# A routed feed-forward kernel in which half a tile of the first expert is placed inside the gating of the last dense tile, and the experts' products hold tokens still

## The reference

```
attention: 8 heads of 64, half of them with a local mask, half with a strided one
dense:     h = x @ w_in (512x2048);  g = h * sigmoid(1.702 h);  x = g @ w_out (2048x512)
routed:    out = x;  rows with x @ w_skip > 0 are computed, the others stay
           e = argmax(x @ w_gate)  (8 experts);  gate = softmax(...)[e]
           out[row] = x[row] + gate * (relu(x[row] @ w1[e]) @ w2[e])   (512x1024, 1024x512)
```

## Time and profile before

| | |
|---|---|
| median of 3 runs | 750.28 us (749.67 to 751.13) |
| profiled execution, its own time | 748.58 us |
| its span, first to last instruction | 747.0 us |
| mean granted TensorE clock | 0.967 of 2.4 GHz |
| TensorE busy | 687.1 us, 92% |
| VectorE, ScalarE, GpSimd busy | 401.9, 355.2, 151.8 us |

### The profile page before, as it was taken

One profiled execution on the slowest core, in us unless ns is written; L12 is line 12 of the kernel. 1 busy time (PEld: TensorE's weight loads), 2 busy tenths in 40 slices (PEclk: granted clock), 3 DMA queues, 4 the chain that ended last, 5 costly groups with the idle time before them and its releaser, 6 DMA issues.

```text
span 747.0 us, 15044 instructions
## 1 busy us (share of the span) xinstructions
PE 687.1 (92%) x4891; PEld 609.6 (82%) x4892; DVE 401.9 (54%) x1401; ACT 355.2 (48%) x1034; POOL 151.8 (20%) x200
## 2 busy tenths in 40 slices
PE   4799999999999999999999999999429999999992
PEld 3578888988888889888988889889329998888882
DVE  4767764474456334243342432523758685668854
ACT  5778765555655333333333332332326563456632
POOL 5345221213223002000010010100240333212331
PEclk9689999999999999999999999999859999999997
DMA  7647633224411502001020020100447686676751
GB/s 255 209 117 259 200 126 98 71 74 145 143 39 65 166 1 85 1 28 59 1 85 0 0 84 0 44 13 1 127 133 229 194 258 204 206 215 181 243 181 43
DMA packets 48455, 85.60 MB, mean 115 GB/s; under 512 B 7858, under 2 KB 11954, under 8 KB 48400
## 3 DMA queue, kind: packets, MB, share of 16 engines
q1 hardware_dynamic: 43664, 79.20, 33.3%
q0 software_dynamic: 3920, 4.65, 2.2%
q10 hardware_dynamic: 816, 1.05, 0.4%
HBM read 70.84 MB, written 18.52 MB: 120 GB/s over the span
## 4 chain that ended last, share of the span: by engine, by line
PE 81%; DVE 5%; issue 5%; ACT 3%; DMA 2%; POOL 2%; SPq 0%; POOLq 0%; DVEq 0%; ACTq 0%
PE px L1199 25%; PE ph L1186 24%; PE pe_h L1296 11%; PE py L1308 9%; PE pscore L1136 3%; PE pctx L1158 2%; PE ptrans L1145 2%; PE ph L1216 2%; PE pxT L1280 1%; PE ph L1210 1%; POOL probs L598 1%; ACT w_hi L705 1%; DMA w_raw<-wf 1%; DMA slot_table<-slot_row,slot_i 1%; DMA xg<-x_dram,gather_slots 1%
## 5 line engine op out<-in xcount | busy, mean ns | idle before, releaser
L994 DVE SCALAR_TENSOR_TENSOR gated<-gated,ph 128x256 f32<-128x256 f32 x144 | 60.6, 421 | 204.8 <-ACT gated L775 203.6
L1186 PE MATMUL ph<-x_hi,w_hi 128*128 128x256 f32 x576 | 165.9, 288 | 0.6 <-DVE x_lo L906 0.6
L1186 PE MATMUL ph<-x_lo,w_hi 128*128 128x256 f32 x576 | 161.1, 280 | 0.0
L1186 PE MATMUL ph<-x_hi,w_lo 128*128 128x256 f32 x576 | 160.9, 279 | 0.0
L1199 PE MATMUL px<-w_hi,g_hi 128*128 128x512 f32 x288 | 119.2, 414 | 0.9 <-DVE g_lo L1003 0.7
L1199 PE MATMUL px<-w_lo,g_hi 128*128 128x512 f32 x288 | 113.9, 396 | 0.0
L1199 PE MATMUL px<-w_hi,g_lo 128*128 128x512 f32 x288 | 113.6, 395 | 0.0
L1186 PEld LDWEIGHTS ph<-x_hi,w_hi 128*128 128x128 f32 x576 | 108.7, 189 | 5.0 <-DVE x_lo L906 0.9
L775 ACT ACTIVATE gated<-ph 128x256 f32<-128x256 f32 x144 | 55.0, 382 | 120.4 <-PE ph L1186 118.2
L1186 PEld LDWEIGHTS ph<-x_lo,w_hi 128*128 128x128 f32 x576 | 108.7, 189 | 4.1
L1186 PEld LDWEIGHTS ph<-x_hi,w_lo 128*128 128x128 f32 x576 | 108.5, 188 | 0.0
(11 more groups left out here) (168 smaller groups left out, 1183.8 us busy)
## 6 DMA issues: line engine op xcount, KB each, us to landing
w_raw<-we SPq DMA_DIRECT2D x72, 256.0 KB
more_raw<-we SPq DMA_DIRECT2D x72, 256.0 KB
w_raw<-wf SPq DMA_DIRECT2D x32, 256.0 KB
vs<-vw SPq DMA_DIRECT2D x16, 384.0 KB, 3.1
qs<-qT SPq DMA_DIRECT2D x16, 288.0 KB, 3.7
ks<-kT SPq DMA_DIRECT2D x16, 288.0 KB, 4.3
xT_dram<-x_stage SPq DMA_DIRECT2D x16, 288.0 KB, 3.2
x_lo<-xT_dram SPq DMA_DIRECT2D x8, 512.0 KB
```

The lines of the kernel that those rows point to most:

```text
L994: nc.vector.scalar_tensor_tensor(gated[s % 2][:, :], gated[s % 2][:, :], 1.0, ph[s % 2][:, 0:TT], ALU.add, ALU.mult).then_inc(gated_done, 1)
L1186: last = nc.tensor.matmul(ph[f % 2][:, 0:TT], up_w(w, k, f), x[p][:, k, :], start=(at == 0 and n == 0), stop=(at == KD - 1 and n == 2))
```

## The change

Three things, in one diff of 825 lines.

1. **The products of the experts keep tokens still.** `e_up(t, p, h, o)` now does one half h (128 slots) and one half o of the hidden columns: the tokens of the half are the stationary operand and 512 columns of weights move. The result has tokens in its partitions, so after the relu the hidden values are transposed on TensorE (`transpose_h`, four per `o`), and the split into `h_hi`, `h_lo` is made from the transposed bank, 128x512 at a time. If a tile has no second half, its `e_up` is skipped too, and dummy matmuls of 96 columns (`idle`) keep the semaphores' counts.
2. **The first half of tile 0 (128 slots of expert 0) runs during the gating of the last dense tile.** Its slots are known before that tile; the gather for them is started from GpSimd inside it. Twelve of expert 0's 16 weight chunks are split in steps 3 to 14 of the last dense tile, into the dense weights' place as it comes free, which gives chunks of parity 0 another order. The pieces of the half's products lie between the transposes, logits and ranks of tile 8.
3. **The second half of tile 0 takes its slots from the chip, not from the table.** VectorE compares each last-tile token's slot with the numbers 128 to 255 (`in_late`), six small matmuls turn that into a list of tokens (`list_late`), and `late_slots` adds what the early table had. GpSimd gathers by it before it scatters the last slots.

With them: the gating's steps move (`T_STEPS` 3, 5, 7, 9 to 2, 3, 4, 5; `LOGIT_STEP` 11 to 6; `RANK_STEP` 14 to 9), `gate_choose` has 5 links of its chain in place of 8, `gate_slots` is cut in `gate_rows`, `gate_slots` and `slots_out`, and some buffers change their place.

```diff
-        T_STEPS = {3: 0, 5: 1, 7: 2, 9: 3}
-        LOGIT_STEP, RANK_STEP = 11, 14
+        T_STEPS = {2: 0, 3: 1, 4: 2, 5: 3}
+        LOGIT_STEP, RANK_STEP = 6, 9
+        def early_chunk(s):
+            return [s - GF + 1] if s >= GF - 1 and s < FB - 1 else []
+        EARLY_CH = FB - GF
...
@@ GpSimd @@
+            pool.wait_ge(slots_stored, 16 * (NT - 1) * TJ)
+            pool.dma_start(gather_slots[0][:, :, :], slot_table[0:ET, :].rearrange("(h p) c -> p h c", p=P)).then_inc(first_slots_in, 16)
+            pool.wait_ge(x2_stored, 32 * (NT - 1))
             pool.wait_ge(first_slots_in, 16)
-            gather(0, 0, 0)
+            gather_first(0, gather_slots[0][:, 0, 0:1])
+            pool.wait_ge(last_x2_stored, 32)
+            pool.wait_ge(late_slots_done, 1)
+            gather_first(1, late_slots[:, 0:1])
+            scatter_slots(NT - 1)
+            pool.wait_ge(slots_stored, 16 * NT * TJ)
...
@@ ScalarE, after the last dense tile @@
+            first_xe_hi(0)
+            copy_x2(NT - 1)
...
+            expert_hi(0, 0, EARLY_CH)
+            relu(0, 0, 0)
+            expert_hi(0, 0, EARLY_CH + 1)
             gate_exp(NT - 1)
+            expert_hi(0, 0, EARLY_CH + 2)
+            relu(0, 0, 1)
+            expert_hi(0, 0, EARLY_CH + 3)
+            split_h_hi(0, 0, 0)
+            split_h_hi(0, 0, 1)
             act.wait_ge(meta_done, 1)
             total = act.value_load(meta[0:1, 3 * T1:3 * T1 + 1], min_val=1, max_val=MAXT)
+            first_xe_hi(1)
...
                 with if_exists(act, total, t):
+                    relu(t, 0, 0)
+                    next_hi(0, 1, 2)
+                    relu(t, 0, 1)
+                    split_h_hi(t, 0, 0)
+                    relu(t, 1, 0)
+                    split_h_hi(t, 0, 1)
+                    next_hi(3, 4, 5)
+                    relu(t, 1, 1)
+                    split_h_hi(t, 1, 0)
+                    next_hi(6, 7, 8, 9, 10)
                     xe_split_hi(t + 1, 1 - p)
+                    split_h_hi(t, 1, 1)
+                    next_hi(11, 12, 13, 14, 15)
...
@@ VectorE, after the last dense tile @@
+            expert_lo(0, 0, EARLY_CH + 2)
+            split_h_lo(0, 0, 0)
+            dve.wait_ge(list_done, 1)
+            nc.vector.tensor_tensor(late_slots[:, :], plist_in(pxT[0]), late_empty[:, :], ALU.add).then_inc(late_slots_done, 1)
+            expert_lo(0, 0, EARLY_CH + 3)
+            split_h_lo(0, 0, 1)
...
+                    split_h_lo(t, 0, 0)
+                    next_lo(0, 1, 2)
+                    split_h_lo(t, 0, 1)
+                    next_lo(3, 4, 5)
+                    split_h_lo(t, 1, 0)
+                    next_lo(6, 7, 8)
                     xe_split_lo(t + 1, 1 - p)
+                    split_h_lo(t, 1, 1)
+                    next_lo(9, 10, 11, 12, 13)
+                    both_rows()
+                    next_lo(14, 15)
...
@@ TensorE @@
-                    for n, (w, x) in enumerate(((w_hi, xe_hi), (w_hi, xe_lo), (w_lo, xe_hi))):
-                        last = nc.tensor.matmul(pe_h[f % 2][:, 0:ET], e_up_w(w, p, k, f), x[p][:, k, :],
+                    for n, (x, w) in enumerate(((xe_hi, w_hi), (xe_hi, w_lo), (xe_lo, w_hi))):
+                        last = nc.tensor.matmul(pe_h[o][:, :], x[p][:, k, h * P:(h + 1) * P], e_up_w(w, p, k, o),
...
+                with pe.If(over > 0):
+                    e_up(t, p, 1, 0)
+                    transpose_h(t, 0, 1)
+                    e_up(t, p, 1, 1)
+                    transpose_h(t, 1, 0)
+                    e_down(t, p, 0, 0)
+                    e_down(t, p, 0, 1)
+                    transpose_h(t, 1, 1)
+                    transpose_xe(t + 1, 1 - p, s + p)
+                    wait(pe, rows_done[1 - p], s + p)
+                    e_down(t, p, 1, 0)
+                    e_down(t, p, 1, 1)
+                with pe.Else():
+                    h_bank_free(t, 1, 0)
+                    idle(pe_h[0]).then_inc(e_up_done, 1)
+                    transpose_h(t, 0, 1)
...
+                    e_down(t, p, 0, 0)
+                    transpose_xe(t + 1, 1 - p, s + p)
+                    e_down(t, p, 0, 1)
...
             all_tiles(pe, tile)
+            first_transposes(0)
             down(NT - 1, FB - 1)
+            e_up(0, 0, 0, 0, range(2))
             for j in range(TJ):
...
+            e_up(0, 0, 0, 0, range(2, KD))
             pe.wait_ge(x2T_copied, (NT - 1) * 2 * TJ + TJ)
...
+            e_up(0, 0, 0, 1, range(KD - 1))
+            gate_ranks(NT - 1, px2[1])
+            e_up(0, 0, 0, 1, range(KD - 1, KD))
+            transpose_h(0, 0, 0)
+            transpose_h(0, 0, 1)
+            list_late()
+            e_down(0, 0, 0, 0)
+            e_down(0, 0, 0, 1)
+            first_transposes(1)
             pe.wait_ge(meta_done, 1)
...
+                with pe.If(over > 0):
+                    e_up(0, p, 1, 0)
+                    e_up(0, p, 1, 1)
+                    transpose_h(0, 1, 0)
+                    transpose_h(0, 1, 1)
+                    e_down(0, p, 1, 0)
+                    e_down(0, p, 1, 1)
...
+                transpose_xe(1, 1 - p, 0)
             def routed_tile(s, p, t):
...
                 with if_exists(pe, total, t):
-                    for f in range(EFB):
-                        e_up(t, p, f)
-                    transpose_xe(t + 1, 1 - p, s + p)
-                    e_down(t, p, 0)
+                    e_up(t, p, 0, 0)
+                    e_up(t, p, 0, 1)
+                    transpose_h(t, 0, 0)
                     second_half(t, s, p)
```

More of the change, by code:

```diff
@@ L61 @@
 NOROW = 1 << 20
+LV = 3
 GW = 96
@@ L789, in tile @@
                         gate_exp(t - 1)
-            all_tiles(act, tile)
-            copy_x2(NT - 1)
+                    if last:
+                        for ch in early_chunk(s):
+                            expert_hi(0, 0, ch)
             def expert_hi(t, p, ch):
@@ new lines, in hT_bank_free, with transpose_h, e_down @@
+            def hT_bank_free(t, h, o):
+                wait(pe, h_lo_done, (t * EH + h - 1) * EFO + o + 1)
+            def transpose_h(t, h, o):
+                pe.wait_ge(relu_done, (t * EH + h) * EFO + o + 1)
+                hT_bank_free(t, h, o)
+                for f in range(FPO):
+                    last = nc.tensor.transpose(phT[o][:, f, :], relu_h[:, o, f * P:(f + 1) * P], ident[:, :])
+                last.then_inc(h_transposed, 1)
+            def e_down(t, p, h, o):
+                if o == 0:
+                    if h == 0:
+                        wait(pe, first_half_done, t)
+                    else:
+                        pe.wait_ge(py_cleared, 1)
+                pe.wait_ge(h_lo_done, (t * EH + h) * EFO + o + 1)
+                for f in range(o * FPO, (o + 1) * FPO):
+                    if h == 0:
@@ L1315, in bank_free @@
                     pe.wait_ge(py_cleared, 1)
                     wait(pe, rows_done[1 - p], s + p)
-                over = pe.value_load(meta[0:1, bass.ds(t + 2 * T1, 1)], min_val=0, max_val=1)
-                with pe.If(over > 0):
-                    bank_free()
-                    e_down(t, p, 1)
-                with pe.Else():
-                    bank_free()
-                    nc.tensor.matmul(py[1][:, 0:GW], ident[:, :], gate_w[:, 0, :], start=True, stop=True).then_inc(e_down_done, 1)
+                    idle(py[1]).then_inc(e_down_done, 1)
@@ new lines, in first_transposes, with list_late @@
+            def first_transposes(h):
+                pe.wait_ge(gathered[0], (h + 1) * 16)
+                for k in range(KD):
+                    last = nc.tensor.transpose(first_pxT(h)[:, k, :], xg[0][:, h, k * P:(k + 1) * P], ident[:, :])
+                last.then_inc(xe_transposed, 1)
+            def list_late():
+                pe.wait_ge(in_late_done, 1)
+                at = [(j, v) for j in range(TJ) for v in range(LV)]
+                for j, v in at:
+                    last = nc.tensor.matmul(plist_in(pxT[0]), in_late[:, j, :], token_parts[:, j, v:v + 1],
+                                            start=((j, v) == at[0]), stop=((j, v) == at[-1]))
+                last.then_inc(list_done, 1)
@@ new lines, in _ @@
+            for step in range(STEPS_ALONE):
+                attention(step)
+            all_tiles(pe, tile)
+            first_transposes(0)
+            down(NT - 1, FB - 1)
+            e_up(0, 0, 0, 0, range(2))
+            for j in range(TJ):
+                pe.wait_ge((x2_copied_a, x2_copied_v)[j], NT)
+                for k in range(KD):
+                    last = nc.tensor.transpose(ph[j][:, k * P:(k + 1) * P], x2[:, j, k * P:(k + 1) * P], ident[:, :])
+                last.then_inc(x2_transposed, TJ)
```

346 lines of the change are left out of this document (213 added, 133 removed).

## The result

| | before | changed |
|---|---|---|
| median | 750.44 us (749.67 to 751.13, 4 runs) | 727.8 us (726.63 to 729.5, 4 runs) |
| ratio of the two | | 0.9699, 95% interval 0.9681 to 0.9717 |
| profiled execution, its span | 748.58, 747.0 us | 726.63, 725.0 us |
| mean granted TensorE clock | 0.967 | 0.991 |

The sign is right, the size is not: the span fell by 22.0 us, not by 13.0.

What follows compares the result with a forecast made beforehand. TensorE, busy 92% of the span, bounds the kernel, with a hole of about 20 us at the gating. 15.1 - 4.5 + 3.3 - 0.9 = 13.0 us less gives a median of 737.3, range 730 to 745.

Steps and rivals of the forecast that it cites:

- Prices: Unit costs: 24 matmuls of 512 columns 5.61 us, eight transposes 0.87; swapping the operands gains nothing by itself.
- The rival of transposes that don't overlap: Added transposes that wait for a relu don't overlap: 17.0 us more, 754 us; three in 100.
- Part 1: Last dense tile: added splits cost 0, moved gating steps 0 (bounds -1 and +1), last `down` 0.8 us late.
- Part 2: TensorE's hole after the last dense product: filled by expert 0's work, tile 1 begins at 567.0, was 582.1; 15.1 us won.
- Part 3: Routed tiles with two halves: 25.2 us each, tiles 2, 3, 4, 6 take 100.8 for 96.3; 4.5 us lost.
- Part 4: Routed tiles with one half: tile 1 17.2 us for 18.0, tile 5 16.2 for 18.7; 3.3 us won.
- (b): One-half tiles are TensorE's: tiles 1 and 5 take 13.8 us, last ends 5 sooner, 11 more gained, 726; 6 in 100.
- Part 5: Last tile, its end set by VectorE: 20.8 to 21.5 us after its start, before 20.4; 0.9 us lost.
- (c): DMA becomes the bound: tiles 1, 5 and 7 take 19.6 us or push the next, 8 lost, 745; 12 in 100.
- (e): Slower: ScalarE stands at `next_hi(2)` for late chunks, 2.6 us lost in each of seven tiles, 755; 5 in 100.
- (d): Early half's rows land 4 us late, shifting the last `down` and the gating behind it: 741 us; 6 in 100.

## Why the prediction was right, and where it failed

**Prices.** Right. 24 matmuls take 5.61 and four transposes 0.44, the chain shows. The rival of transposes that don't overlap is out: 16 of them in a two-half tile make 1.75 us together, 0.109 each, with the relu ahead of them. The Trainium skill, TensorE: Matmul & The Clock Gate, Part 4: PE-mode transpose, gives about 275 ns for one; that is the duration of one, and the step from one to the next is what a row of them costs.

**Part 1 is the step that failed most**, with 4.1 of the 9.0 us: "The moved gating steps contain the same work as before less three links; 0, bounds -1 and +1 over eight tiles." The work is the same, but where it stood the gating met the split of the next tile's input on VectorE. Beside attention the slots' scatter then held GpSimd, and TensorE waited 2.3 us for GpSimd's `probs`; in the loop `g_lo` came late. Moved, it gains 4.7 us in the dense stage. Some 2.3 of them are lost again in the changed kernel, as they are in the kernel before when unused buffers shift the others. In the profiled pair another 1.1 us lies in the time up to the end of tile 0, by which executions of one kernel differ too (106.0 to 107.4 in three traces of the changed kernel); that part is chance. The other half of Part 1, that `down` starts 0.8 late, fell too: the early rows are there when the transposes come, these end at 523.53, and `down` starts at 523.55.

**Part 2, the hole.** The steps and their order were right: meta done 17.5 us after the last `down` (20.7 forecast), the second half's product after 19.8 (22.0), tile 1 after 35.3 (37.6). The step that failed is "Now 18 matmuls (4.2) stand ahead of the ranks": three of the four blocks of the contraction by three products are 9 matmuls, 2.1 us. Behind the ranks it has "six matmuls 1.4", where one block is left, three matmuls. With the two groups of six that makes 36 matmuls, and the prediction's own price of this product is 24: 12 too many, 2.8 us, which is nearly all of the 3.2 by which meta came early. The nine end about when the experts are chosen, and the ranks come 0.6 us after `chosen_b`. The half costs the gating 1.5 us instead of over 4. A part of that came back: from the end of meta to the product are 2.3 us, where 1.3 were put. The clock stayed at 1.00, as forecast. By undoing parts, the early products are worth 9.3 us, the late list in place of the table 7.0, both with the early gather 21.6.

**Part 3.** 25.2 forecast, 25.0 to 25.1 measured. Before, 23.7 to 24.6 of it held 0.4 to 1.3 us of waits that other chips don't show; against a tile of 23.3 without them the price of two halves is 1.75 us, the 16 transposes.

**Part 4.** Tile 1 came out at 17.4 (17.2 forecast; 17.1 in two other traces), and in part by luck. ScalarE did wait for chunks that were not there yet, 1.6 us in all, as forecast. But of the 2.5 us that TensorE stood idle 1.5 were for the gathered rows of tile 2, which the forecast of this tile doesn't have. Tile 5 was put at 16.2 because VectorE has 15 us of work in it. It does, but it begins the work 6.8 us into the tile and finishes it 6.7 us into the next one, whose TensorE has work enough; the tile takes 14.9, near what rival (b) gave for TensorE alone (13.8). The bound of an engine over one tile was right for the load of a row of such tiles and too high for a single one between two-half tiles.

**Part 5.** The last rows end 20.3 us after the tile's start, a little under the 20.8 to 21.5 forecast; that VectorE's order sets it is shown by the rows moved ahead of five chunks, 3.1 us earlier.

**The rivals.** (c) and (e) didn't come: the DMA share is 0.83 in tile 1 and at most 0.76 in the tiles after, and in no two-half tile does TensorE wait for a chunk. (d) didn't come. (b) gave 726, near the 727.8 measured, but that nearness is chance: of its 11 us 1.3 came in tile 5 and 1.0 in the last tile, and the rest of the miss is the dense stage and the 12 matmuls counted too many. The range was too narrow below because Part 1 was bounded at -1, by the idea that work that is the same costs the same in another step; the chain in the tiles beside attention has VectorE and GpSimd in it, and it was there to be read.

## What to carry to other kernels

Ask of work that is moved what it stood beside, not only whether it is the same: follow the chain through one tile of each kind before you put a moved step at nothing. Count the instructions of a product once as a whole and once by its pieces; the two must agree. A dependence that goes through memory (store, load, indirect gather) is best broken by working out the one value that is late on the chip and by having independent work of the right length beside it; here that paid twice, in the wait and in the clock after it. An engine's sum over one tile bounds that tile only if its neighbours are as full; count how much may spill into the next. And in orders that are written by hand, an operation brought forward delays the splits behind it and with them the loads that they release.

## What the runs showed of the hardware

- The same matmuls took 1.43 us a dozen where they took 1.40, only because unused buffers had shifted the others (11.52 and 11.21 us for a routed up product).
- The same product of 24 matmuls behind a gap of about 2.5 us on TensorE went at full speed in five executions (in one of them 5.84 us behind 2.50 us, granted clock 1.00) and at a lower clock in a sixth, with the dummy moved: 7.35 us behind 2.48 us, granted clock 0.76. Behind 1.98 us it took 7.36 us at 0.77.
- One kernel differed by 5 us in 750 from chip to chip through waits of under a microsecond each, while its variant without those waits didn't. What causes them, and why addresses matter, stays open.
